# Two attention contractions split into column halves of TensorE, on one core of Trainium2

## The reference

```python
def phi(x):
    proj = np.einsum('bhsd,df->bhsf', x, w_phi)                       # 128 features
    proj = proj - np.max(np.abs(proj), axis=-1, keepdims=True)
    return np.concatenate([np.exp(proj), np.exp(-proj)], axis=-1)     # 256 features
q_p, k_p = (phi(q), phi(k))
kv = np.einsum('bhsf,bhsd->bhfd', k_p, v)          # contraction over tokens
z = np.sum(k_p, axis=2)
num = np.einsum('bhsf,bhfd->bhsd', q_p, kv)        # contraction over features
den = np.einsum('bhsf,bhf->bhs', q_p, z)[..., None] + 1e-06
out = num / den
```

## Time and profile before

| | |
|---|---|
| median of 3 runs | 902.22 us |
| profiled execution | 901.18 us, its span 899.6 us |
| TensorE matmuls (PE) | 884.7 us busy, 98% of the span, 6242 records |
| weight loads (PEld) | 874.0 us busy, 97%, 6242 records |
| VectorE, ScalarE, GpSimd | 374.0, 292.5 and 101.2 us busy |
| mean granted TensorE clock | 0.995 of full speed |

### The profile page before, as it was taken

One profiled execution on the slowest core, in us unless ns is written; L12 is line 12 of the kernel. 1 busy time (PEld: TensorE's weight loads), 2 busy tenths in 40 slices (PEclk: granted clock), 3 DMA queues, 4 the chain that ended last, 5 costly groups with the idle time before them and its releaser, 6 DMA issues.

```text
span 899.6 us, 14982 instructions
## 1 busy us (share of the span) xinstructions
PE 884.7 (98%) x6242; PEld 874.0 (97%) x6242; DVE 374.0 (42%) x641; ACT 292.5 (33%) x581; POOL 101.2 (11%) x67
## 2 busy tenths in 40 slices
PE   8999999999999999999999999999999999999997
PEld 7899999999999999999999999999999999999997
DVE  5565574365763467733794442122122122122111
ACT  3545454345642355423542331111211111111111
POOL 5541121000210002100240001010010010010000
PEclk8999999999999999999999999999999999999999
DMA  7999612327322093042572621201201201201001
GB/s 184 271 265 244 188 55 76 84 72 252 102 80 81 21 292 94 1 165 91 191 240 100 197 72 36 71 1 36 71 1 36 71 1 36 71 1 36 36 1 35
DMA packets 106033, 88.96 MB, mean 99 GB/s; under 512 B 61040, under 2 KB 92656, under 8 KB 103920
## 3 DMA queue, kind: packets, MB, share of 16 engines
q1 hardware_dynamic: 105216, 87.82, 32.8%
q10 hardware_dynamic: 752, 0.20, 0.1%
HBM read 70.18 MB, written 17.83 MB: 98 GB/s over the span
## 4 chain that ended last, share of the span: by engine, by line
PE 88%; DVE 7%; issue 3%; ACT 2%; POOL 0%; ACTq 0%; DVEq 0%
PE kvb L1110 8%; PE qnb L1053 7%; PE qnb L1054 7%; PE qnb L1055 7%; PE qnb L1140 7%; PE pjb L1053 6%; PE pjb L1055 5%; PE pjb L1054 5%; PE mb L1053 5%; PE mb L1055 5%; PE mb L1054 5%; PE tpb L1053 2%; PE kvb L1055 2%; PE tpb L1054 2%; PE kvb L1053 2%
## 5 line engine op out<-in xcount | busy, mean ns | idle before, releaser
L974 DVE SCALAR_TENSOR_TENSOR c_lo<-qnb,c_hi 128x384 fp32r<-128x384 f32 x94 | 52.4, 558 | 282.6 <-ACT c_hi L751 282.6
L751 ACT ACTIVATE c_hi<-qnb 128x384 fp32r<-128x384 f32 x94 | 46.3, 492 | 294.2 <-PE qnb L1055 290.3
L1053 PE MATMUL qnb<-u_hi,w_b 128*128 128x384 f32 x384 | 129.8, 338 | 0.0
L1055 PE MATMUL qnb<-u_hi,w_b 128*128 128x384 f32 x384 | 128.4, 334 | 0.0
L1054 PE MATMUL qnb<-u_lo,w_b 128*128 128x384 f32 x384 | 128.4, 334 | 0.0
L520 POOL TENSOR_TENSOR g_lo<-cv,g_hi 128x576 fp32r<-128x576 f32 x31 | 46.2, 1491 | 344.8 <-DVE g_hi L793 344.8
L1053 PEld LDWEIGHTS qnb<-u_hi,w_b 128*128 128x128 f32 x384 | 72.1, 188 | 0.1
L1054 PEld LDWEIGHTS qnb<-u_lo,w_b 128*128 128x128 f32 x384 | 72.2, 188 | 0.0
L1055 PEld LDWEIGHTS qnb<-u_hi,w_b 128*128 128x128 f32 x384 | 72.1, 188 | 0.0
L808 DVE TENSOR_REDUCE nm<-pjb 128x4 f32<-128x512 f32 (+1 forms) x80 | 50.6, 632 | 46.7 <-PE pjb L1055 46.4
L1053 PE MATMUL mb<-x_hi,winr 128*128 128x288 f32 x224 | 69.3, 309 | 0.0
(11 more groups left out here) (254 smaller groups left out, 1916.5 us busy)
## 6 DMA issues: line engine op xcount, KB each, us to landing
winr<-wi_dram SPq DMA_DIRECT2D x32, 512.0 KB, 4.2
woutr<-wo_dram SPq DMA_DIRECT2D x15, 1024.0 KB, 5.3
stage<-in_moe_w_ch_dram SPq DMA_DIRECT2D x32, 256.0 KB, 4.0
us<-u_dram SPq DMA_DIRECT2D x6, 768.0 KB, 4.8
ua<-u_dram SPq DMA_DIRECT2D x6, 768.0 KB, 4.7
qr<-in_q_dram SPq DMA_DIRECT2D x32, 128.0 KB, 2.7
vt<-in_v_dram SPq DMA_DIRECT2D x32, 128.0 KB, 3.2
wi_dram<-aw SPq DMA_DIRECT2D x8, 512.0 KB, 5.6
```

The source lines that it names most:

```text
L751: nc.scalar.activation(c_hi[:, j % CR, :], CH[j % 2][:, 0:TW], ACT.Relu).then_inc(s_chh, 1)
L974: nc.vector.scalar_tensor_tensor(out=c_lo[:, j % CR, :], in0=CH[j % 2][:, 0:TW], scalar=0.0, in1=c_hi[:, j % CR, :].bitcast(F32), op0=ALU. ...
L1053: mm(o, a_hi, b_hi, start=start, stop=False)
L1055: return mm(o, a_lo, b_hi, start=False, stop=stop)
```

## The change

Each product of `contract_k`, and each of `contract_q` except those of the tail, is written as two: the first with stationary columns 0 to 63 into partitions 0 to 63 of the output, the second with columns 64 to 127 into partitions 64 to 127. Both have the same moving operand. The tail's product has 64 stationary columns where it had 66, and goes into partitions 0 to 63. The program gives such a product another shape and place in the array: 128 rows by 64 columns, at column 0 or 64, where it gave 128 by 128 at column 0 before. The order of the calls and every wait stay as they are, and so do the instructions of the other engines.

```diff
+            def halves(o, a, b, start, stop):
+
+                for m in range(0, P, P // 2):
+                    last = mm(o[m:m + P // 2], a[:, m:m + P // 2], b, start=start, stop=stop)
+                return last
+
...
                     for s in range(2):
-                        last = mm(KV[:, s, h, :],
-                                  feat_t[:, h, s, :] if u == TL else feat[:, u, n, s, :],
-                                  vt[:, g % 2, h, TM if u == TL else 2 * u + tt, :],
-                                  start=(u == K0 and n + s == 0), stop=(u == TL and n + s == 2))
+                        last = halves(KV[:, s, h, :],
+                                      feat_t[:, h, s, :] if u == TL else feat[:, u, n, s, :],
+                                      vt[:, g % 2, h, TM if u == TL else 2 * u + tt, :],
+                                      start=(u == K0 and n + s == 0), stop=(u == TL and n + s == 2))
...
-                    rows = slice(0, TAIL + 2 if t == TM else P)
                     a = t * P - HALF[half][0]
                     for h in range(2):
                         for s in range(2):
-                            last = mm(NUM[rows, h, token_slot(t), :], qf[:, half, s, h, a:a + rows.stop],
-                                      kvf[:, g % 2, s, h, :], start=(t + s == 0), stop=((t, s) == (TM - 1, 1)))
+                            o, kvs = NUM[:, h, token_slot(t), :], kvf[:, g % 2, s, h, :]
+                            if t == TM:
+                                mm(o[QROWS], qf[:, half, s, h, a:a + TAIL], kvs, start=False, stop=False)
+                            else:
+                                last = halves(o, qf[:, half, s, h, a:a + P], kvs,
+                                              start=(t + s == 0), stop=((t, s) == (TM - 1, 1)))
```

## The result

The changed kernel takes 880.51 us (median of 4 runs, 879.79 to 881.36), the kernel before 901.68 us in the runs beside it (899.07 to 903.17): a ratio of 0.977, 95% interval 0.975 to 0.979. It is 21 us faster. I had forecast 936 us. The time is near rival A, to which I gave 0.28 and 875 us.

What follows compares the result with a forecast made beforehand. TensorE, busy 98% of the span, was taken to bound the kernel. 901.2 us plus 38.2 for more records and division changes, less 3 hidden by waits, gave 936 us; own range 924 to 945, 8-in-10 range 872 to 945.

Steps and rivals of the forecast that it cites:

- rival A: In the contractions, two halves load and multiply side by side, 60 ns a pair, visits still paid: 875 us, chance 0.28.
- What bounds the kernel: Whole run: TensorE, busy 98% of the span, sets the time, except for a few microseconds near the start.
- Part one: In the contractions, 1152 whole products become 2304 halves, 120 ns a pair against 112 ns: 9.2 us more.
- The other end of my bound: In the contractions, halves load and multiply side by side, 60 ns a pair, saving 59.9 us.
- Part two: At each contraction stretch, the array's division changes to 64 columns and back, draining TensorE: 0.34 us for each visit.
- a visit: One stretch of products in another array division, entered and left again: taken as 0.34 us, 72 stretches in all.
- The sum: Over all 72 contraction stretches: 38.2 us more, less 3 us hidden by waits, giving 936 us.
- What I named to look at: Inside a stretch of the changed profile: 32 records in 1.9 us for the forecast, about 1.0 us for side by side.
- The granted clock: In the contractions: it should stay at 1.00, the 2.4 GHz level.
- The waits for ACT and DVE: On TensorE: growth beyond the present 4.5 us, although TensorE is slower, would show the summed forecast wrong.
- The chances: Whole kernel: forecast itself 0.54; slower 0.66, same 0.02, faster 0.32.

Runs made afterwards that it cites:

- experiment 3: The changed kernel with whole products and the 66-column tail in the ticks ahead of the gated network, halves only from there on: 879.21 us.
- Experiment 1: The changed kernel with, in each call, all half products into columns 0 to 63 first, then all into 64 to 127: 912.94 us.
- Experiment 2: The kernel before with only the tail's products cut from 66 to 64 stationary columns: 905.65 us, ratio 1.0051.
- experiment 7: The changed kernel with the contraction over features moved next to that over tokens, only in each batch's twelve ticks with hidden channels: 875.85 us.
- experiment 4: The changed kernel with four quarters of 32 stationary columns in place of two halves of 64, the tail in two: 889.21 us.
- experiment 5: The changed kernel with the eight write-backs of prepared weights two ticks earlier in SyncE's order: 878.63 us.

## Why the prediction was wrong

Point by point, by its own steps.

**What bounds the kernel** was right for the part from 100 us on and too kind for the first. I read 6.9 us of idle time there as the only slack. The profile had more to say: the DMA share of the first 100 us is 0.92, and PE's first product of the network stood at 85.37 us without a wait only because the weights had landed 1.0 us earlier, at 84.36. A faster TensorE could hardly move that start, as the changed kernel's wait of 5.8 us and experiment 3 show.

**Part one is the step that failed**: "if they follow one another as now, two halves cost 120 ns where one whole costs 112", and its choice, "I take the 9.2 us, the value of the row that shows one 66-column product after another". That row shows products in the same columns of the array, one after another. The change makes neighbours in different columns, and those run side by side, loads and matmuls both: a pair costs 58 ns. The other end of my bound, 60 ns for a pair, was the right one. My reason for the choice was that in every row a load begins when the matmul ahead of it begins. That is so where both use the same columns, and says nothing where they don't. The row that I wanted did not exist in the trace, and I filled the gap with the nearest one as if the nearest were the likelier. Experiment 1 puts it right: with the same halves in the order in which my row applies, the kernel is 12 us slower than before.

Where two pages of the Trainium skill were divided, the runs decide. TensorEngine Tiling (Array Packing), section Tiling Modes, says that tiles can load weights and multiply in parallel; the trace agrees, with 58 ns for two and for four. The Trainium skill's other page, TensorE: Matmul & The Clock Gate, says in Part 3 that a load overlaps matmuls in flight only where the row group differs; that does not hold here, as both halves use all 128 rows and their loads still start 7 ns apart.

**Part two held.** I took 0.34 us for a visit and 0.05 for the load that the first record no longer hides. Experiment 2 gives 0.28 (0.20 to 0.37), experiment 7 gives 0.31: the mechanism is right, and its size was somewhat too large. The Trainium skill's rule on the change of tiling mode, which I had quoted from TensorEngine Tiling (Array Packing), section Tiling Modes, agrees with this for a division by columns too.

**The sum.** Behind 85 us there are 34 stretches of 16 records, 12 of 24 and 11 of 8. From the single records, from the matmul ahead of a stretch to the third behind it, I read 2.185 us before and 1.679 after for 16 records, 2.643 and 2.117 for 24, and 1.289 and 1.212 for 8. That makes 34 x 0.506 + 12 x 0.526 + 11 x 0.077 = 24.4 us. From the network's first product to the start of the last contraction the records show 333.96 us before and 313.14 after, 20.8 less. Two things account for most of the 3.6 us between. PE's idle time behind the start of the network rose from 2.7 to 4.4 us (the length less the busy time in the middle rows above), 1.6 us more. And the first products of the network ran at the 1.2 GHz level, behind the wait of 5.8 us:

```profile
85.72:88.65 2.93, 2.93 (x12) 2.93 (x13) 0.00 (x0) 0.00 (x0) 0.00 (x0) 0.50 1.24 242
```

The first 20 take 4.07 us where they took 2.74, 1.3 us more. That leaves 0.7 us open. Rival A's own sum, 26 us, had 5 us too much from the first 85 us, where I left it half of the joined stretches and it got none. The rest of it, 20.6 us, meets the measured 20.8 partly by luck: its stretches gave too little (the visit is cheaper than 0.34 us, the pitch is 58 and not 60 ns), and it had nothing for the waits and the clock that took 3.6 us back. The short stretches of 8 records are nearly a draw, as it said.

**What I named to look at** did its work: 32 records in about 1.0 us stood there as the sign of A. The granted clock was said to stay: behind 88.7 us it is 1.00 to the end of the contractions. Ahead of the network the mean fell from 0.96 to 0.92, with stretches at the 1.2 GHz level around TensorE's waits (the first product behind the wait of 5.8 us shows 0.61 us where 0.38 is usual). The waits for ACT and DVE I had named as a sign against the sum; they did grow (4.5 us became 6.7 with the 1.6 us for high and low parts of the queries), and with them waits for DMAs that I had not named at all.

**The chances.** Forecast 0.54 against A 0.28 was a guess between two readings that the trace could not tell apart, and the text says so ("the trace decides neither"). With that said, even odds would have been the honest ones. A slower kernel was forecast and a faster one came, so the range of 872 to 945 us holds the time only because it was drawn to hold rival A.

## What to carry to other kernels

Products whose pace is set by the load of the stationary operand (here 128 columns, with 66 moving ones: 112 ns a record) can be cut by columns into two that stand next to each other in the order. Such pairs run side by side, 58 ns a pair here, and a finer cut gave nothing more. Each visit to another division of the array cost about 0.3 us, so put such products next to each other in long stretches (here a stretch of eight records barely pays), but look first what chain a moved piece was covering. And before counting a gain in the first part of a kernel, look for the first product that needs data prepared in that part: if it starts at the same time whatever is faster, the gain stays there.

## What the runs showed that I had not expected

- TensorE takes a product for free columns ahead of earlier ones for busy columns, a few places ahead: three pairs in the stretch of experiment 1 (1.83 us instead of 2.0), and the product at 295.55 us of the changed kernel.
- Four quarters run side by side as two halves do: 64 records in 1.06 us.
- More instructions for TensorE can cost time by their own transfer. With quarters nine gaps, 12.7 us in all by their single lengths, end 1.2 to 1.5 us after a block of 16 KB of instructions has landed, six of them in the part with a DMA share of 0.9. With halves there is none of this kind in the changed kernel's trace, and one of 0.5 us in experiment 5's.
- "issue" in the waits is a name for two different things here: gaps at a block of instructions (experiment 4) and gaps that end 0.09 us after a load of values landed (1.5 us in the changed kernel). The times of the landings tell them apart.
